# Attention in blocks of 32 queries and 64 keys, five TensorE steps a batch, the first batch's transfers on two queues

## The reference

```python
mask_local = (rel >= 0) & (rel < 32)
mask_strided = (rel >= 0) & (pos[None, :] % 32 == pos[:, None] % 32)
scores = np.where(masks, scale * q @ k.T, -1e9)
attn = np.exp(scores - max); attn = attn / (attn.sum(-1) + 1e-09)
out = attn @ v
```

## Time and profile before

| | |
|---|---|
| median of 3 runs | 704.28 us (704.14 to 705.2) |
| profiled execution | 704.93 us |
| its span | 703.2 us |
| mean granted TensorE clock | 0.963 |

### The profile page before, as it was taken

The page is one execution under the profiler, slowest core; times in us unless marked ns, Lnnn a source line. Parts: engine busy times, 40 slices in busy tenths (PEclk is TensorE's granted clock), DMA queues, the critical chain, the costliest instruction groups (busy, mean ns, idle before and its releaser), DMA issues.

```text
span 703.2 us, 11023 instructions
## 1 busy us (share of the span) xinstructions
PE 657.1 (93%) x4149; PEld 567.4 (81%) x4149; DVE 330.2 (47%) x614; ACT 229.0 (33%) x693; POOL 149.3 (21%) x163
## 2 busy tenths in 40 slices
PE   7999892299999999989999999999999999999995
PEld 4877762299999999968888888888888888888994
DVE  3877733032111112387445644456445564455653
ACT  4999932032111111122223322233222332222331
POOL 1655506302221222785000200002000020000201
PEclk8999977599999999999999999999999999999998
DMA  8565166693777776222000100001000010000100
GB/s 259 180 214 207 40 255 261 225 394 126 265 263 248 262 264 225 88 94 60 1 1 0 61 1 0 1 0 60 0 0 0 0 60 0 0 0 1 61 1 30
DMA packets 37854, 73.95 MB, mean 105 GB/s; under 512 B 2739, under 2 KB 16224, under 8 KB 37808
## 3 DMA queue, kind: packets, MB, share of 16 engines
q1 hardware_dynamic: 34936, 63.92, 26.3%
q0 software_dynamic: 2880, 9.52, 3.5%
HBM read 63.49 MB, written 9.94 MB: 104 GB/s over the span
## 4 chain that ended last, share of the span: by engine, by line
PE 82%; ACT 6%; DMA 4%; POOL 3%; issue 2%; DVE 2%; SPq 0%; DVEq 0%
PE pair L970 28%; PE pair L983 15%; PE bank L983 12%; PE pair L927 10%; PE bank L937 9%; ACT prob L489 5%; DMA WE<-w 2%; POOL x_sorted L418 2%; PE bank L841 1%; PE bank L827 1%; PE bank L911 1%; PE pair L814 1%; PE bank L868 1%; DMA k_loc<-kT 1%; ACT XT L497 1%
## 5 line engine op out<-in xcount | busy, mean ns | idle before, releaser
L970 PE MATMUL pair<-yh,WIH 128*128 128x512 f32 (+1 forms) x320 | 116.5, 371 | 0.2 <-ACT yh L548 0.2
L970 PE MATMUL pair<-yh,WIL 128*128 128x512 f32 (+1 forms) x320 | 116.3, 370 | 0.0
L572 ACT ACTIVATE cl<-cl,half 128x512 f32<-128x512 f32 (+1 forms) x80 | 54.5, 681 | 187.2 <-DVE cl L768 187.2
L477 POOL DMA_INDIRECT out<-XT,tok x18 | 18.8, 1045 | 351.6 <-DVE XT L756 347.7
L776 DVE TENSOR_TENSOR gl<-gr,gh 128x512 fp32r<-128x512 f32 (+1 forms) x80 | 56.3, 703 | 73.1 <-ACT gh L581 71.9
L768 DVE TENSOR_SCALAR cl<-pair 128x512 f32<-128x512 f32 (+1 forms) x80 | 50.9, 637 | 71.0 <-PE pair L970 70.8
L970 PE MATMUL pair<-yl,WIH 128*128 128x512 f32 (+1 forms) x320 | 79.9, 370 | 2.1 <-DVE yl L747 2.1
L927 PE MATMUL pair<-xw,WE 128*128 128x168 f32 x512 | 75.7, 310 | 0.3 <-DMA WE<-w 0.3
L927 PEld LDWEIGHTS pair<-xw,WE 128*128 128x128 f32 x512 | 74.5, 193 | 0.7 <-DMA WE<-w 0.6
L581 ACT CAST gh<-gr 128x512 fp32r<-128x512 f32 (+1 forms) x80 | 46.3, 578 | 85.7 <-PE bank L983 58.3
L937 PE MATMUL bank<-hid,WE 128*128 128x168 f32 x512 | 74.1, 306 | 0.0
(11 more groups left out here) (124 smaller groups left out, 933.7 us busy)
## 6 DMA issues: line engine op xcount, KB each, us to landing
WE<-w SPq DMA_DIRECT2D x16, 2048.0 KB, 9.1
xrow<-x_sorted SPq DMA_DIRECT2D x6, 781.5 KB, 10.5
raw_in<-win SPq DMA_DIRECT2D x16, 256.0 KB, 9.2
raw_out<-wout SPq DMA_DIRECT2D x16, 256.0 KB, 2.5
v_loc<-vl SPq DMA_DIRECT2D x4, 768.0 KB, 5.1
q_str<-qT SPq DMA_DIRECT2D x4, 576.0 KB, 5.8
k_str<-kT SPq DMA_DIRECT2D x4, 576.0 KB, 6.8
q_loc<-qT SPq DMA_DIRECT2D x3, 576.0 KB, 4.6
```

Source lines behind the costliest of these rows:

```text
L477: pool.indirect_dma_start(out, bass.IndirectOffsetOnAxis(tok[:, GT * g + t:GT * g + t + 1], 0), rows_of(g, t), None).then_inc(out_done if ...
L572: act.activation(cl[:, 0:n], cl[:, 0:n], ACT.Square, bias=half[:, :], scale=0.5).then_inc(squared, 1)
L970: last = pe.matmul(h2_b[f % 2][:, 0:tokens], w[:, c, P * f:P * (f + 1)], x[:, c, 0:tokens], start=(k == 0), stop=(k == 3 * DC - 1))
```

## The change

A batch is now cut by 64 keys. The strided heads' positions make strips of 54 queries (three classes) with 64 keys; two strips lie over each other in the 128 rows, and two such tiles side by side make the steps "strips A" and "strips B". The local heads' positions make blocks of 32 queries with 64 keys, four over each other and two side by side, in the steps "blocks A" and "blocks B". What is left of a batch (one strip, one block and one single class on each side) makes the rest step. So there are 5 steps a batch and 20 in all, each with 8 groups of 64 columns on 128 rows. Queries and keys of a batch are each loaded in one transfer for each kind of head; values come in three buffers. For the first batch SyncE issues `q_str`, `q_loc`, `v_str`, `v_rest` and ScalarE `k_str`, `k_loc`, `v_loc`.

VectorE subtracts the maximum and writes the result to SBUF; ScalarE takes one exponential of 128x512; VectorE sums it. ScalarE copies the transposed weights. A strip step has 16 matmuls for scores and 16 for values, the rest step 24 and 24, a block step 32 and 32; each step has 4 mask matmuls of 128 columns and 4 transposes of 128x128. The order on TensorE is: transposes of n, scores of n+3, values of n; the rest step's scores are done in two halves around the transposes. VectorE, GpSimd and ScalarE have no loop any more, TensorE's loop holds five rounds. The second part of the constants, the gate's weights and the padding rows are transferred in batches 1 and 2.

```diff
-LQ = 96
-CLASSES = [6, 6, 5, 5, 5, 5]
-TWINS = [(TILES[i], TILES[i + 1]) for i in range(0, len(TILES), 2)]
+BLOCK, KEYS = 32, 64
+BLOCKS = S // BLOCK
+STRIP = 3 * PHASE
+PAIR = 2 * STRIP
+FIRST_BLOCKS = [t for t in range(BLOCKS) if t % 4 in (1, 2) and t < BLOCKS - 2]
+Part = namedtuple("Part", "row kind first queries keys store index out step")
+def strip(w, j, x):
+    out, step, store, index = (STRIP * x, PAIR, "str", w) if w < STRIP_PAIRS - 1 else (0, STRIP, "rest", 0)
+    return Part(KEYS * x, "s", PAIR * w + PHASE + STRIP * j, STRIP, PAIR * w + PHASE + STRIP - KEYS + KEYS * j, store, index, out, step)
+def block(t, j, n):
+    return Part(BLOCK * n, "l", BLOCK * t, BLOCK, BLOCK * (t - 1), "loc", FIRST_BLOCKS.index(t - 2 * j), BLOCK * n, P)
+def rest_of_batch(j):
+    t, c, out = (BLOCKS - 1) * j, (STRIDE - 1) * j, STRIP * 2
+    return [strip(STRIP_PAIRS - 1, j, 0),
+            Part(KEYS, "l", BLOCK * t, BLOCK, max(0, BLOCK * (t - 1)), "rest", 1, out, BLOCK),
+            Part(KEYS + BLOCK, "s", PHASE * c, PHASE, (S - KEYS) * j, "rest", 2, out + 2 * BLOCK, PHASE)]
+STRIPS_A, STRIPS_B, REST_STEP, BLOCKS_A, BLOCKS_B = range(5)
+SCORES_IN = [0, 1, 2, 0, 1]
+SLOTS = TB
+LAG = FIRST = 3
+LOOPS = (STEPS - FIRST) // TB
...
 SyncE
-            load_local(0, q1=2 * LQ, k1=2 * LQ, arrived=qk_first_in)
-            load_local(0, q0=2 * LQ, k0=2 * LQ)
-            load_v_local(0)
-            sp.dma_start(con[:, C_UP:C_END], cst[:, C_UP:C_END]).then_inc(con_in, 16)
-            load_strided(0)
+            sp.dma_start(q_str[:, :, :], qT[0, 1]).then_inc(qk_str_in, 16)
+            sp.dma_start(q_loc[:, :, :], qT[0, 0]).then_inc(qk_loc_in, 16)
             load_v_strided(0)
+            load_v_rest(0)
+            for b in range(1, B):
+                done = TB * (b - 1)
+                sp.wait_ge(scored, done + REST_STEP + 1)
+                load_qk_strided(b)
+                if b > 1:
+                    sp.wait_ge(pv_done, done)
+                    load_v_local(b - 1)
+                sp.wait_ge(scored, done + TB)
+                load_qk_local(b)
+                sp.wait_ge(pv_done, done + STRIPS_B + 1)
                 load_v_strided(b)
+                sp.wait_ge(pv_done, done + REST_STEP + 1)
+                load_v_rest(b)
+                if b == 1:
+                    sp.dma_start(con[:, C_UP:C_END], cst[:, C_UP:C_END]).then_inc(con_in, 16)
...
+            sp.wait_ge(pv_done, TB * (B - 1))
+            load_v_local(B - 1)
...
 GpSimd
-                for j in range(2):
-                    pool.tensor_tensor(pr, pr, inv.unsqueeze(3).to_broadcast([q, 2, 2, kk]), ALU.mult).then_inc(normed, 1)
+            for n in range(STEPS):
                 pool.wait_ge(inverted, n + 1)
+                pool.tensor_tensor(weights, weights, sm[:, n % SLOTS, 24:32].unsqueeze(2).to_broadcast([P, 8, KEYS]), ALU.mult).then_inc(normed, 1)
...
 ScalarE
-                for e in range(8):
-                    last = act.activation(prob[0:q, i % 3, e * kk:(e + 1) * kk], score_b[i % 2][0:q, e // 4, e % 4 * kk:(e % 4 + 1) * kk], ACT.Exp,
-                                          bias=sm[0:q, i % 3, 8 + e:9 + e], scale=SCALE, accum_out=sm[0:q, i % 3, 16 + e:17 + e])
+            act.dma_start(k_str[:, :, :], kT[0, 1]).then_inc(qk_str_in, 16)
+            act.dma_start(k_loc[:, :, :], kT[0, 0]).then_inc(qk_loc_in, 16)
+            act.dma_start(v_loc[:, :, :], vl[0, :, 0:LOC]).then_inc(v_loc_in, 16)
+            def exps(n):
+                act.wait_ge(lowered, n + 1)
+                act.activation(prob[:, n % SLOTS, :], prob[:, n % SLOTS, :], ACT.Exp, scale=SCALE).then_inc(probs_done, 1)
+            def copy_turned(n):
+                act.wait_ge(turned, n + 1)
+                behind(act, pv_done, n)
+                act.copy(probT[:, :], probT_b[:, :]).then_inc(turn_copied, 1)
+            def place(n):
+                b, i = divmod(n, TB)
+                act.wait_ge(pv_done, n + 1)
...
+            for s in range(STEPS + LAG):
+                if 0 <= s - 1 < STEPS:
+                    exps(s - 1)
+                if 0 <= s - LAG < STEPS:
+                    copy_turned(s - LAG)
+                    place(s - LAG)
...
 VectorE
+            def maxima(n):
+                dve.wait_ge(scored, n + 1)
+                behind(dve, normed, n - SLOTS + 1)
+                dve.tensor_reduce(small[:, 0:8].rearrange("q (h g) -> q h g", h=2), scores, AX_X, ALU.max).then_inc(maxed, 1)
+                dve.wait_ge(maxed, n + 1)
+                behind(dve, turned, n - SLOTS + 1)
+                dve.tensor_tensor(prob[:, n % SLOTS, :].rearrange("q (h g k) -> q h g k", g=4, h=2), scores,
+                                  small[:, 0:8].rearrange("q (h g) -> q h g", h=2).unsqueeze(3).to_broadcast([P, 2, 4, KEYS]), ALU.subtract).then_inc(lowered, 1)
+            def inverses(n):
...
+                dve.tensor_reduce(small[:, 8:16], prob[:, n % SLOTS, :].rearrange("q (g k) -> q g k", g=8), AX_X, ALU.add).then_inc(summed, 1)
+                dve.tensor_scalar(small[:, 16:24], small[:, 8:16], 1e-9, None, ALU.add).then_inc(guarded, 1)
+                dve.reciprocal(small[:, 24:32], small[:, 16:24]).then_inc(inverted, 1)
+            for s in range(STEPS + 1):
+                if s < STEPS:
+                    maxima(s)
+                if s >= 1:
+                    inverses(s - 1)
...
 TensorE
+            def scores_of(i, hh):
+                for j, (mask, _) in enumerate(TILES_OF[i]):
+                    pe.matmul(out.rearrange("q (p j k) -> q p j k", p=2, j=2)[:, :, j], ident_b[:, :], mask_b[:, mask, :].unsqueeze(1).to_broadcast([P, 2, KEYS]), ...)
+                for j, (_, parts) in enumerate(TILES_OF[i]):
+                    for p in range(2):
+                        for x in parts:
+                            yield pe.matmul(out[x.row:x.row + x.queries, col:col + KEYS], queries[half_, p, x.first:x.first + x.queries], keys[half_, p, x.keys:x.keys + KEYS], ...)
+            def scores(n, i, b):
+                await_scores(n, i, b)
+                for _, last in zip(scores_of(i, 0), scores_of(i, 1)):
+                    pass
+                last.then_inc(scored, 1)
+            def turn(n, i):
+                pe.wait_ge(normed, n + 1)
+                for g in range(4):
+                    last = pe.transpose(probT_b[:, P * g:P * (g + 1)], prob[:, i, P * g:P * (g + 1)], ident)
+                last.then_inc(turned, 1)
+            def values(n, i, b):
+                pe.wait_ge(turn_copied, n + 1)
+                for p in range(2):
                     for hh in range(2):
+                        for pair in zip(*(parts for _, parts in TILES_OF[i])):
+                            for j, x in enumerate(pair):
+                                last = pe.matmul(out_b[KEYS * hh:KEYS * (hh + 1), j, to:to + x.queries], vv[half_, x.index, HD * h:HD * (h + 1)],
+                                                 probT[half_, from_:from_ + x.queries], start=True, stop=True)
                 last.then_inc(pv_done, 1)
+            def round_of(n, i, b, later, scoring):
+                m, k, c = later
+                if not scoring:
+                    turn(n, i)
+                elif k == REST_STEP:
+                    half_scores(m, k, c, 0)
+                    turn(n, i)
+                    half_scores(m, k, c, 1)
+                else:
+                    turn(n, i)
+                    scores(m, k, c)
+                values(n, i, b)
```

More of the change, by code:

```diff
@@ L1 @@
+import itertools
+from collections import namedtuple
 from contextlib import ExitStack
@@ L246, in behind, with x_strided @@
                 eng.wait_ge(signal, value)
[L248 to L256, removed]
+        def x_strided(b):
+            return XT[:, 2:4, S * b:S * (b + 1)].rearrange("d p (m r) -> d p r m", r=STRIDE)
         @block.sync
@@ L615, in copy_turned @@
-            def copy_turned(n, i):
-                behind(dve, pv_done, n)
-                for j in range(2):
-                    q, kk, _, _, _, _ = TWINS[i][j]
-                    dve.wait_ge(turned, 2 * n + j + 1)
-                    dve.tensor_copy(probT[0:kk, j, 0:4 * q], probT_b[j][0:kk, 0:4 * q]).then_inc(turn_copied, 1)
-            def step(k, s, b):
-                for lag, work in ((LAG, copy_turned), (0, maxima), (1, inverses)):
-                    m = s - lag
-                    if isinstance(m, int) and not 0 <= m < STEPS:
-                        continue
-                    work(m, (k - lag) % TB)
@@ L845, in step @@
-            def step(k, s, b):
-                for lag, work in ((LAG, turn), (0, scores), (LAG, values)):
-                    m = s - lag
-                    if isinstance(m, int) and not 0 <= m < STEPS:
-                        continue
-                    work(m, (k - lag) % TB, b + (k - lag) // TB)
-            steps(pe, step, LAG)
+            def scores_of(i, hh):
+                out = score_b[SCORES_IN[i]][:, hh, :]
```

(19 more changed lines are left out.)

266 lines of the change are left out of this document (123 added, 143 removed).

## The result

The changed kernel takes 714.94 us (median of 4 runs, 711.59 to 716.29), the kernel before 704.74 in the runs beside it. The ratio is 1.0137, 95% interval 1.0099 to 1.0174: slower, by 1.4%. The recorded execution is the fastest of the four: 711.59 us, span 709.6, mean granted clock 0.939.

What follows compares the result with a forecast made beforehand. ScalarE and TensorE, both nearly full, were taken to bound the attention. Start 17.5, four batches of 17.4, less 3.95 and 0.7, plus 3 x 0.8 and 2.3, gave 87.2 for 92.99 us: 698.5 us, range 685 to 716.

Steps and rivals of the forecast that it cites:

- rival of dear small matmuls: TensorE's score and value runs in block steps: records cost 27 to 40 ns, kernel slower, 705 to 725 us; chance 0.28.
- values of step 0 start: Attention's start: first transfers in by 7.6 us, product at 14.2, step 3's 64 records end at 16.6 to 18.5; taken 17.5.
- three batches (17.4 + 0.8 each): Attention's batches: step intervals sum to 17.4 us for 19.32 before, plus 0.8 a batch for changes of tile width.
- from there to the router: Last batch: 17.4 us less 3.95 (step 19 without interval) and 0.7 (step 18 without scores ahead), plus 2.3 for the tail.
- Small records: TensorE's score and value matmuls: 22 ns a record, bounds 13 (four tiles overlap) to 40, deciding from about 26.
- The loop without the rest step's scores: Attention's rounds: interval is values plus the larger of ScalarE's part and TensorE's (1.13 us plus scores of n+4).
- The loop over VectorE and GpSimd: From scores n+3 to the turn of n+2: 3.95 us where rounds leave 3.94 or more, at its edge.
- I take 0.8: Rest step's scores on TensorE: 16 changes of tile width cost 0 to 1.6 us a batch, taken as 0.8.
- My upper bound from the gaps between runs: Changes of tile width on TensorE: at most 0.10 us each, 1.6 us a batch.
- The clock: Rival: TensorE idles some 0.7 us in strip rounds, clock falls from 2.4 to 1.2 GHz, over 725 us; chance 0.08.
- The title's second part: First batch's transfers, keys and local values issued on ScalarE's queue: alone worth 1 to 2 us.
- my last rival: Whole kernel: nothing moves, only if records cost just 26 ns; the first batch's transfers alone give 1 to 2 us; chance 0.03.

Runs made afterwards that it cites:

- split32_busy: Changed kernel with the rest step's 54 queries cut into 32 and 22, plus unread 512-column matmuls where TensorE would idle: 691.18 us, ratio 0.9805.
- after_busy: Changed kernel, widths 54, 32, 18 kept, plus unread 512-column matmuls at the attention's start and end: 705.93 us, ratio 1.0025.
- grouped: Changed kernel with each half of the rest step's scores ordered all 54-wide matmuls first, one width change a half: 704.92 us, ratio 0.9999.
- by_side: Changed kernel with each half of the rest step's scores sorted by width within each side, three width changes a half: 707.21 us, ratio 1.0041.
- split32: Changed kernel with the rest step's 54 queries multiplied as 32 and 22, no output wider than 32: 697.23 us, ratio 0.9887.
- before_busy: Kernel before the change plus unread 512-column matmuls behind the first three steps' scores and the last two steps' transposes: 702.69 us, ratio 0.9958.

## Why the prediction was wrong

It forecast 698.5 us and faster; the time is 714.94, slower. That lies inside its range (685 to 716) and inside the 705 to 725 of its rival of dear small matmuls, by luck: that rival's mechanism is refuted below. In spans, where it expected 697.4 (703.2 less 5.8), the trace has 709.6. The 12.2 us between them, by the forecast's own marks (the three batches run from 21.81 to 82.52 us):

| part | forecast | measured | difference |
|---|---|---|---|
| values of step 0 start | 17.5 | 21.81 | 4.3 |
| three batches (17.4 + 0.8 each) | 54.6 | 60.71 | 6.1 |
| from there to the router | 15.1 | 16.15 | 1.1 |
| router | 6.77 | 7.44 | 0.7 |

**Small records: dearer in the forecast than on the chip.** I took 22 ns, near 20 for scores and 24 for values. Measured by starts: scores 10 ns in block steps and 14 in strips, values 20, 18 and 17 (1.46, 1.05 and 0.73 us for 64, 48 and 32, less 0.22). This was the term with the widest bounds and the heaviest rival, and the rival at 27 to 40 ns is refuted. The trace disagrees, too, with the floor of about 25 ns that the Trainium skill has (TensorE: Matmul & The Clock Gate, section Wait — 56ns, not 53.3ns?), at least for records that take turns over several parts of the array.

**The loop without the rest step's scores: right, and a little better.** The interval of strips A takes 2.94 us (forecast 3.24), of strips B 2.70 (3.00), of the rest step 2.96 (3.31). The two behind them hold the loss: blocks A, with the scores of the next rest step, 6.39 (3.90 and 0.8 for the widths), blocks B 4.96 (3.95). The exponential's hold, the copies, VectorE's 2.7 us and the transfers in batches 1 to 3 of the changed kernel were as costed; the exponential's row is some 635 ns. The loop over VectorE and GpSimd is at its edge, as forecast: at full clock, in split32_busy, TensorE waits 0.20 us for GpSimd's product.

**The rest step's scores: mis-sized.** "I take 0.8" for 16 changes of width a batch, and at most 1.6. Measured 0.12 us each, 1.7 us for the 14 inside the halves. Beside that its records were costed at 22 ns like all others, but the 54-wide ones of a half go one by one at about 57. Together the two halves take 3.76 us at full clock; the forecast's terms for them (1.06 + 0.30 + 0.8) make 2.16. The rule that I weighed, that a change of the tiling mode drains the engine (the Trainium skill, TensorEngine Tiling (Array Packing), Key Properties), agrees with the trace in that every change costs time; that the engine drains, no trace shows. My upper bound from the gaps between runs was still too low.

Inside the batches this alone would not have cost the sign. The batch of after_busy at full clock has all these changes and takes 17.66 us against my 17.4 + 0.8, since the other rounds were shorter than forecast, and against 19.32 before. Three batches at full clock tell the two parts of the price: 17.66 us with seven changes a half (after_busy), 16.18 with one (grouped, 48.32 to 64.50), 15.25 with none and 32 + 22 in place of 54 (split32_busy). So 1.5 us a batch are the changes, and 0.9 are what the wide records, one behind the other, cost beyond the narrow ones.

**The clock: the step that failed.** I gave its fall 0.08 and put it into the strip rounds, "the idle is in pieces below 1 us and rounds stay over 70% busy". The strip rounds do keep 1.00. The clock falls in the rest step's scores, where TensorE starts only 14 records in a microsecond and its row shows no pause, and stays at 0.50 for about 6 us, until 63: over the rest of the second half, the values of blocks B (2.4 us where 1.41 was costed; those of blocks A run before the fall, in 1.46), the transposes (1.04 for 0.59), the scores of blocks A and the values of strips A. It does so in each of the three batches. They take 60.71 us where three at 17.66 would take 53.0: 7.7 us for a term that the sum had at nothing, less 1.6 by which 17.66 is under 18.2, make the 6.1 of the table. In the recorded execution these 7.7 us turn a gain of 1.3 us in the span into a loss of 6.4. It is the fastest of the four, 3.4 us below their median, and after_busy with its clock held in two of three batches is no faster than the kernel before. So the clock is the largest failed term; that it alone turned the sign of the median is not shown.

Four kernels cross the two causes. Medians, in us (they come from different sessions, in which the kernel before took 704.3 to 705.2):

| | as they are | with extra matmuls |
|---|---|---|
| widths 54, 32, 18 | 714.94 | 705.93 |
| 32 and less | 697.23 | 691.18 |

The extra matmuls bring 9.0 us in the upper row and 6.1 in the lower, some 2.9 of each in the router (7.44 and 7.38 us to 4.50); cutting the 54 to 32 + 22 brings 17.7 and 14.8. The extra matmuls alone bring the kernel before 2.5 (705.23 to 702.69). So the 54-wide records among narrow ones cost about 2.4 us a batch directly (17.66 less 15.25), 9.6 in four. That the rest came through the clock is an inference: it fits grouped and by_side, where the clock holds with shorter halves, but the fall was never set apart from the length of the halves.

**The start: one thing in front of another.** My transfer was near: first scores at 8.71 us for 7.6, inside its range. VectorE's and GpSimd's part then ended at 15.38 (GpSimd's product starts at 14.34), near my 14.2. But I let the transposes follow at once. TensorE works in order, and the rest scores of step 2 stand before them: q_loc arrives at 12.33, the two halves take 2.97 and 2.93 us at clock 0.50, and the transposes start at 19.04, 3.7 us after the product is ready. The order alone costs nothing: split32 has it too, its halves are short, and its transposes start at 14.99, right behind the product, and values at 17.64. So this is the rest step's scores a second time, at half clock. I named what is queued on ScalarE and VectorE there, and not what is queued on TensorE.

**The title's second part** is worth nothing that can be measured, or a little less; the "1 to 2 us" of my last rival did not show.

What stays open: what causes the stops without a releaser, why keys of a later batch sometimes land 7 to 8 us after their issue, and why the clock falls in one batch and not in the next with the same instructions. The best kernel, split32_busy, is 2% faster than the kernel before; before_busy, with such matmuls alone, is 0.4% faster.

## What to carry to other kernels

Do not mix output widths from different tile sizes within a run of small matmuls: sort them, or cut the wide ones down to the narrow tile even if that makes more instructions. Cost a run of small matmuls not only by its own length but by what the granted clock does behind it, and look for the fall in stretches with few records as well as in idle ones. When a step is moved ahead of another on an in-order engine, ask of the first round too what stands before it in the queue.

## What was not expected of the hardware

- A change between 54-wide and 32-wide outputs costs 0.12 us at full clock (halves of 1.14, 1.39 and 1.88 us with 1, 3 and 7 changes).
- TensorE can lose its clock in a stretch that its row calls busy throughout: 1.00 to 0.50 around 57 us, the last pause 5 us back, in a run that starts 14 records a microsecond.
- Small f32 records start 10 ns apart (block scores, eight tiles in turn) or 14 (strip scores, four), but 57 where all use one part of the array.
- TensorE stops of 0.9 to 3.7 us without a releaser, more of them in the two kernels with the longer instruction stream (17 instruction packets in 100 us for 9).
